# Retention with its batches' chunks in turn, its state in a ring of its own, and the first expert's layer in sixteen half tiles

## The chip, the cores and the metric

The kernel runs on one core of one Trainium2 chip. The metric is the device time of one execution in microseconds (us); a smaller number is better. Engines are named as in the profile: PE is TensorE (PEld its weight load), DVE VectorE, ACT ScalarE, POOL GpSimd, SP SyncE; a q behind a name is the queue of that engine.

## The reference, cut to what matters

Three parts follow each other. The first is a causal retention with a decay for each head, the second a mixture of 4 experts with all tokens through every expert, the third an MLP with a mish activation, which the kernel treats as experts 4 and 5.

```python
batch, n_heads, seq, head_dim = (2, 8, 576, 64)
scores = scale * np.matmul(q, k.transpose(0, 1, 3, 2))
gamma = 1.0 - 2.0 ** (-5.0 - np.arange(H, dtype=np.float32))
Dmat = np.where(rel >= 0, gamma[:, None, None] ** rel[None, :, :], 0.0)
ret = scores * Dmat[None, :, :, :]
attn = np.matmul(ret, v)                       # (2, 8, 576, 64) -> x (1152, 512)
for e in range(4):                             # w1 (512, 1024), w2 (1024, 512)
    out += p[:, e:e + 1] * (np.maximum(x @ w1[e], 0.0) @ w2[e])
g = h * np.tanh(softplus(h))                   # h = out @ w_in (512, 2048)
result = g @ w_out                             # (1152, 512)
```

## The kernel before

Retention works on 18 chunks of 64 tokens, nine for each batch, all nine of batch 0 first. A chunk lies in one of six slots of `qkv`: v and k by keys on partitions 0 to 63, k and q by features on partitions 64 to 127. For chunk c PE computes the scores of 8 heads (L448, rows 64 to 127 of the array, columns 0 to 63) and adds k times v of the chunk to the running state (L452, rows 0 to 63, columns 64 to 127): the two are issued head by head in turn and lie on opposite quarters of the array. `masked` on DVE (L822) writes the masked scores over k, POOL's `v_decay` (L1025) multiplies v in place with its decay, `state_copy` on ACT (L696, two pieces) writes the state over the next chunk's k by features, and `output` (L488) multiplies both with 128 rows at once. `decayed` on DVE (L837) takes the output out of bank 3, `first_hi` on ACT (L702) and `first_lo` on DVE (L843) split it in two fp32r parts. Since the next chunk is of the same batch, the state of chunk c has to be copied before `output(c + 1)`, and before the next state matmuls of its half (a wait inside L461).

The order on PE is written out by hand in 19 turns. Turn c holds the scores of chunk c + 1 and the state of c, then the output of chunk c - 1. The first expert's layer 1 for the first 384 tokens (8 tiles, banks 6 and 7, waits in `plain_ready`) is cut in 16 halves of two contraction steps, 6 matmuls of 384 columns each (L494 to L496). Before, a half stands behind the scores of turns 8 to 18 and another behind the output of turns 7 to 11. Matmuls on zeros (`keep_warm`, L626) stand at the start (9), behind the first scores (5) and in turns 0 (3) and 6 (8).

```python
WARM = 9
WARM_IN = {0: 3, 6: 8}
```

The weights of the experts are split by jobs: `job_hi` on ACT (L368; L364 for the sums of weight blocks, kind "s") and `job_lo` on POOL (L395; L382 to L390 for "s"). IN_TURN says in which turn a job stands; raw weights come in a ring of 8 buffers. SP issues the loads of chunks and weights in a written order with waits between them (`load_chunk`, `chunk_there`, `load_weights`). Constants come in two further loads, one on SP's queue, one on ACT's.

Behind the turns comes layer 2 of the first stage, `second(0, q)` for q from 0 to 11 with three matmuls each; it takes unit q // 3 of w2. From there on PE follows a fixed list of products and second-layer pieces for all experts, which the change doesn't touch.

## Time and profile before

| what | us |
|---|---|
| median of 3 runs | 626.67 |
| lowest and highest run | 625.93, 629.63 |
| span of the profiled execution | 625.2 |
| PE busy in that span | 618.1 |
| DVE, ACT, POOL busy | 271.6, 237.0, 285.0 |

The profiled execution is known by its span, from its first to its last instruction; the median of the runs stands 1.47 us above that. The busy time of PE is counted from modelled ends of pipelined matmuls. A few per cent of the matmul records can be missing.

### The profile page before, as it was taken

Reading aid. Unit: us, or ns where it says so; the run is one execution under the profiler, and the core shown is the slowest. Engines: PE = TensorE matmul, PEld = TensorE weight load, DVE = VectorE, ACT = ScalarE, POOL = GpSimd, SP = SyncE. Lnnn points to the kernel's source line nnn. Section 1 sums busy time; section 2 is a strip of 40 time slices with the busy share of each in tenths; the row PEclk is TensorE's granted clock in tenths of the full one; section 3 lists DMA queues with packets and bytes.
Section 4 is the critical chain, followed back from the end, with each engine's and each line's share of the span. In section 5 each row is a group of like instructions: output and inputs, shape, how many; then the busy total and the mean of one; then the engine's idle time right before and its main releaser. Section 6 shows DMA issues by size and latency. Waiting matters only on the chain.

```text
span 625.2 us, 9507 instructions
## 1 busy us (share of the span) xinstructions
PE 618.1 (99%) x3773; PEld 553.7 (89%) x3773; DVE 271.6 (43%) x388; ACT 237.0 (38%) x459; POOL 285.0 (46%) x239
## 2 busy tenths in 40 slices
PE   8999999999999999999999999999999999999997
PEld 5788899999999999999999899988989999989996
DVE  5646854433154433154433154434545432324334
ACT  3446423432223432123442223435455454334431
POOL 4657645553435542535543635532435553443300
PEclk9999999999999999999999999999999999999999
DMA  8955312332102321212312212321211233201002
GB/s 271 318 185 174 106 48 68 101 89 63 51 35 68 102 79 57 68 35 67 102 67 69 69 35 67 88 81 35 68 34 35 68 117 85 68 0 52 1 0 102
DMA packets 25147, 50.43 MB, mean 81 GB/s; under 512 B 2896, under 2 KB 3216, under 8 KB 25104
## 3 DMA queue, kind: packets, MB, share of 16 engines
q1 hardware_dynamic: 24816, 49.66, 25.4%
q8 instruction: 31, 0.51, 0.3%
q10 hardware_dynamic: 288, 0.17, 0.1%
q14 instruction: 12, 0.10, 0.0%
HBM read 47.45 MB, written 2.36 MB: 80 GB/s over the span
## 4 chain that ended last, share of the span: by engine, by line
PE 97%; DMA 1%; DVE 1%; issue 0%; ACT 0%; SPq 0%; DVEq 0%; ACTq 0%
PE bank L494 31%; PE bank L496 30%; PE bank L495 30%; PE bank L448 2%; PE bank L488 2%; DMA qkv<-in_chunks 1%; PE bank L619 1%; PE bank L452 1%; PE bank L626 0%; DVE acc_sb L895 0%; DVE acc_sb L899 0%; ACT qkv L696 0%; DVE qkv L822 0%; DVE h_lo L856 0%; SPq L418 0%
## 5 line engine op out<-in xcount | busy, mean ns | idle before, releaser
L395 POOL TENSOR_TENSOR w_lo<-w_raw,w_hi 128x512 fp32r<-128x512 f32 x96 | 132.2, 1389 | 150.7 <-ACT w_hi L368 148.9
L494 PE MATMUL bank<-w_hi,h_hi 128*128 128x512 f32 x432 | 168.8, 391 | 0.0
L496 PE MATMUL bank<-w_hi,h_lo 128*128 128x512 f32 x432 | 168.4, 390 | 0.0
L495 PE MATMUL bank<-w_lo,h_hi 128*128 128x512 f32 x432 | 168.3, 390 | 0.0
L882 DVE TENSOR_TENSOR h_act<-part,bank 128x384 f32<-128x384 f32 x96 | 52.9, 552 | 169.7 <-PE bank L496 168.9
L390 POOL TENSOR_TENSOR ws<-ws_f,ws 128x1024 fp32r<-128x1024 f32 x24 | 57.6, 2400 | 145.1 <-ACT ws L364 145.1
L496 PEld LDWEIGHTS bank<-w_hi,h_lo 128*128 128x128 f32 x432 | 81.1, 188 | 16.9
L495 PEld LDWEIGHTS bank<-w_lo,h_hi 128*128 128x128 f32 x432 | 81.1, 188 | 12.3
L494 PEld LDWEIGHTS bank<-w_hi,h_hi 128*128 128x128 f32 x432 | 81.0, 188 | 12.2
L732 ACT ACTIVATE part<-bank 128x384 f32<-128x384 f32 x72 | 35.4, 491 | 139.3 <-PE bank L496 139.3
L849 DVE SCALAR_TENSOR_TENSOR h_lo<-h_act,h_hi 128x384 fp32r<-128x384 f32 x64 | 74.3, 1170 | 20.6 <-ACT h_hi L722 20.0
L494 PE MATMUL bank<-xa_hi,w_hi 128*128 128x384 f32 x192 | 66.4, 346 | 0.0
L496 PE MATMUL bank<-xa_hi,w_lo 128*128 128x384 f32 x192 | 64.5, 336 | 0.0
L495 PE MATMUL bank<-xa_lo,w_hi 128*128 128x384 f32 x192 | 64.4, 336 | 0.0
L856 DVE TENSOR_TENSOR h_lo<-h_act,h_hi 128x384 fp32r<-128x384 f32 x48 | 38.2, 797 | 55.5 <-ACT h_hi L727 55.1
L368 ACT ACTIVATE w_hi<-w_raw 128x512 fp32r<-128x512 f32 x96 | 57.2, 618 | 0.0
L722 ACT ACTIVATE h_hi<-h_act 128x384 fp32r<-128x384 f32 x64 | 33.5, 525 | 58.5 <-DVE h_act L882 58.5
L495 PE MATMUL bank<-xt,ws 128*128 128x384 f32 x144 | 48.4, 336 | 0.0
L496 PE MATMUL bank<-xt,ws 128*128 128x384 f32 x144 | 48.4, 336 | 0.0
L494 PE MATMUL bank<-xt,ws 128*128 128x384 f32 x144 | 48.4, 336 | 0.0
L849 DVE SCALAR_TENSOR_TENSOR h_lo<-bank,h_hi 128x384 fp32r<-128x384 f32 x32 | 17.7, 554 | 59.9 <-ACT h_hi L713 59.9
L713 ACT ACTIVATE h_hi<-bank 128x384 fp32r<-128x384 f32 x32 | 15.7, 491 | 73.7 <-PE bank L496 73.7
(87 smaller groups left out, 911.4 us busy)
## 6 DMA issues: line engine op xcount, KB each, us to landing
w_raw<-in_weights SPq DMA_DIRECT2D x144, 256.0 KB, 2.8
qkv<-in_chunks SPq DMA_DIRECT2D x18, 512.0 KB, 4.6
out<-acc_sb SPq DMA_DIRECT2D x6, 256.0 KB, 2.0
out<-acc_sb SPq DMA_DIRECT2D x1, 768.0 KB, 3.6
consts<-in_consts ACTq DMA_DIRECT2D x1, 146.0 KB, 3.6
ident<-in_consts SPq DMA_DIRECT2D x1, 64.0 KB, 4.0
consts<-in_consts SPq DMA_DIRECT2D x1, 34.0 KB, 3.9
p_nat<-in_probs ACTq DMA_DIRECT2D x1, 18.0 KB, 3.6
```

Of the source, the lines that this page charges most:

```text
L368: act.activation(w_hi[int(kind == "w2")][:, x], w_raw[:, r % RAW], ACT.Copy).then_inc(s_wh, 1)
L390: pool.tensor_tensor(w_sum(x)[:, 1], ws_f[:, :], w_sum(x)[:, 0].bitcast(F32), ALU.subtract)\
L395: pool.tensor_tensor(w_lo[layer][:, x], w_raw[:, r % RAW], w_hi[layer][:, x].bitcast(F32), ALU.subtract).then_inc(s_wl, 1)
L494: pe.matmul(out, w[0], x[0], start=first, stop=False, **more)
L495: pe.matmul(out, w[0], x[1], start=False, stop=False, **more)
L496: return pe.matmul(out, w[1], x[0], start=False, stop=last, **more)
L713: act.activation(h_hi[:, tile_slot(s, i)], banks[6 + i % 2][:, 0:TC], ACT.Relu).then_inc(s_hh, 1)
L722: act.activation(h_hi[:, tile_slot(s, i)], h_act[:, i % 2], ACT.Relu).then_inc(s_hh, 1)
L732: act.activation(part[:, i], banks[6][:, 0:TC], ACT.Copy).then_inc(s_pt, 1)
L849: dve.scalar_tensor_tensor(h_lo[:, slot], full, 0.0, h_hi[:, slot].bitcast(F32), ALU.max, ALU.subtract).then_inc(s_hl, 1)
L856: dve.tensor_tensor(h_lo[:, slot], h_act[:, i % 2], h_hi[:, slot].bitcast(F32), ALU.subtract)\
L882: dve.tensor_tensor(h_act[:, i % 2], part[:, kept], banks[bank][:, 0:TC], op).then_inc(s_cc, 1)
```

## The change

Chunks alternate between the batches: chunk c is of batch c % 2 and at place c // 2 in it. Each batch has a state of its own, in bank 4 or 5. The decayed v and the copied state no longer go into `qkv` but into `sv`, a ring of four, so `state_copy` is one instruction and serves the chunk two further on. The outputs of chunks 0, 2 and 4 go to bank 6, the others to bank 3. Constants and chunk 0 come in one load on SP's queue. Weights are loaded from behind chunk 7 on. The matmuls on zeros are 7 at the start and 3 behind the first scores, and none in the turns. The sixteen halves all stand behind the output, in turns 7 to 17, in five of these turns two at a time, and the jobs' turns are written out anew. `first_lo` comes one turn later. Outside the kernel the tokens' rows are put back in order; the tables of constants are changed to match.

```diff
--- before.py
+++ after.py
...
+SLOT = 2 * HEADS * CH
+RING = 4
+
+
+def batch(c):
+    return c % BATCH
+
+
+def place(c):
+    return c // BATCH
 
 
 def has_state(c):
-    return c % PER_BATCH < PER_BATCH - 1
+    return place(c) < PER_BATCH - 1
...
-AFTER_SCORES = {8: (0, 1), 9: (1, 1), 10: (2, 1), 11: (3, 1), 12: (4, 1), 13: (5, 0), 14: (5, 1),
-                15: (6, 0), 16: (6, 1), 17: (7, 0), 18: (7, 1)}
-AFTER_OUTPUT = {7: (0, 0), 8: (1, 0), 9: (2, 0), 10: (3, 0), 11: (4, 0)}
-HIDDEN_IN = {t: c for c, (t, half) in AFTER_SCORES.items() if half}
-
-ROWS_IN = {0: 4, 1: 5, 6: 6, 7: 7, 8: 8}
-
-
-WARM_IN = {0: 3, 6: 8}
+
+
+
+HALVES_IN = {7: (0,), 8: (1, 2), 9: (3,), 10: (4,), 11: (5, 6), 12: (7, 8), 13: (9,), 14: (10, 11), 15: (12,),
+             16: (13, 14), 17: (15,)}
+ENDS_IN = {turn: half // 2 for turn, halves in HALVES_IN.items() for half in halves if half % 2}
+JOBS_IN = {6: (("w1", 0, 0),), 7: (("w1", 0, 1),), 8: (("w1", 0, 2),), 9: (("w1", 0, 3),), 10: (("w2", 0, 0),),
+           11: (("w1", 0, 4),), 12: (("w1", 0, 5),), 13: (("w2", 0, 1),), 14: (("w1", 0, 6),), 15: (("w1", 0, 7),),
+           16: (("w2", 0, 2),), 17: (("s", 0, 0),), 18: (("w2", 0, 3), ("w2", 0, 4), ("w2", 0, 5))}
+
+ROWS_IN = {5: 4, 9: 5, 11: 6, 13: 7, 15: 8}
+WARM_START, WARM_NEXT = 7, 3
...
-    for u in range(UNITS):
-        add(IN_TURN, 5 + u, "w1", 0, u)
-    for u in range(3):
-        add(IN_TURN, 12 + u, "w2", 0, u)
-    add(IN_TURN, 15, "s", 0, 0)
-    for u in range(3, 6):
-        add(IN_TURN, 13 + u, "w2", 0, u)
+    for turn, jobs in JOBS_IN.items():
+        for job in jobs:
+            add(IN_TURN, turn, *job)
...
+        sv = sb("sv", [P, RING, HEADS, DH])
...
-        ps_s = [banks[i][KEYS, :].rearrange("p (h c) -> p h c", h=HEADS) for i in range(SCORES)]
-        ps_state = [banks[i][FEATS, 0:HS * DH].rearrange("p (h c) -> p h c", h=HS) for i in range(2)]
-        ps_o = banks[3][:, 0:PAIRS * CH].rearrange("p (h c) -> p h c", h=PAIRS)
+        by_pairs = [bank[:, 0:PAIRS * CH].rearrange("p (h c) -> p h c", h=PAIRS) for bank in banks]
+        by_heads = [bank[:, :].rearrange("p (h c) -> p h c", h=HEADS) for bank in banks]
+        ps_s = [bank[KEYS] for bank in by_heads[0:SCORES]]
+        ps_state = [bank[FEATS] for bank in by_heads[4:4 + BATCH]]
...
+        def ps_o(c):
+
+            return by_pairs[6 if c < PER_BLOCK and c % 2 == 0 else 3]
...
-            load_chunk(0)
-            sp.dma_start(consts[KEYS, 0:ROW0], consts_in[KEYS, 0:ROW0]).then_inc(s_const, 16)
+            sp.dma_start(loaded[:, lead - CONSTS:lead + SLOT], first_in).then_inc(s_slot[0], 16)
             load_chunk(1)
-
-            for c in range(2, 6):
-                if c > 2:
-                    chunk_there(c - 3)
-                load_chunk(c)
-            for u in range(UNITS):
-                chunk_there(3 + u)
-                load_weights(u)
-                chunk_there(4 + u)
-                load_chunk(6 + u)
-            for c in range(6 + UNITS, CHUNKS):
+            load_chunk(2)
+            for c in range(3, 8):
                 chunk_there(c - 3)
                 load_chunk(c)
-                load_weights(UNITS + c - 6 - UNITS)
-            sp.dma_start(ident[:, :], consts_in[:, CONSTS:]).then_inc(s_id, 16)
-            for r in range(UNITS + CHUNKS - 6 - UNITS, len(LOADS)):
+            for c in range(8, CHUNKS):
+                chunk_there(c - 2)
+                load_weights(c - 8)
+                load_chunk(c)
+            sp.dma_start(ident[:, :], ident_in).then_inc(s_id, 16)
+            for r in range(CHUNKS - 8, len(LOADS)):
...
-                return pe.matmul(ps_state[h // HS][:, h % HS], by_keys(c, 1)[:, h], by_keys(c, 0)[:, h],
-                                 start=(c % PER_BATCH == 0 and h % HS == 0), stop=True, skip_group_check=True)
+                return pe.matmul(ps_state[batch(c)][:, h], by_keys(c, 1)[:, h], sv[KEYS, c % RING, h],
+                                 start=(place(c) == 0 and h == 0), stop=True, skip_group_check=True)
...
+                    if place(c) > 0:
+                        pe.wait_ge(s_st, states(c - BATCH))
                 for h in range(HEADS):
-                    if has_state(c) and c > 0 and h % HS == 0:
-                        pe.wait_ge(s_st, 2 * states(c - 1) - 1 + h // HS)
...
-                if c % PER_BATCH > 0:
+                if place(c) > 0:
                     rows = slice(0, P)
-                    pe.wait_ge(s_st, 2 * states(c - 1))
-                if c > 0:
+                    pe.wait_ge(s_st, states(c - BATCH))
+                if c >= PER_BLOCK:
                     pe.wait_ge(s_xt, c)
+                elif c > 1:
+                    pe.wait_ge(s_xt, c - 1)
                 for hp in range(PAIRS):
                     for x in range(2):
-                        mm = pe.matmul(ps_o[DH * x:DH * (x + 1), hp], qkv[rows, c % SLOTS, 0, 2 * hp + x],
+                        mm = pe.matmul(ps_o(c)[DH * x:DH * (x + 1), hp], sv[rows, c % RING, 2 * hp + x],
                                        qkv[rows, c % SLOTS, 1, 2 * hp + x], start=True, stop=True)
...
-            keep_warm(WARM)
+            keep_warm(WARM_START)
             pe.wait_ge(s_slot[0], landed(0))
             for h in range(HEADS):
                 mm = scores_head(0, h)
             mm.then_inc(s_sc, 1)
-            keep_warm(5)
+            keep_warm(WARM_NEXT)
             for c in range(TURNS):
                 if c < CHUNKS:
                     scores_and_state(c)
-                if c in AFTER_SCORES:
-                    plain_half(*AFTER_SCORES[c])
-                keep_warm(WARM_IN.get(c, 0))
                 if c > 0:
                     output(c - 1)
-                if c in AFTER_OUTPUT:
-                    plain_half(*AFTER_OUTPUT[c])
+                for half in HALVES_IN.get(c, ()):
+                    s, i = divmod(half // 2, ITEMS)
+                    if half % 2 == 0:
+                        plain_ready(s, i)
+                    plain_products(s, i, range(KH * (half % 2), KH * (half % 2 + 1)))
...
-                act.wait_ge(s_sc, c + 2)
+
                 act.wait_ge(s_kv, states(c))
-                for i in range(2):
-                    at = by_feats(c + 1, 0)[:, HS * i:HS * (i + 1)]
-                    act.activation(at, ps_state[i], ACT.Copy).then_inc(s_st, 1)
+                if c >= BATCH:
+                    act.wait_ge(s_o, c - BATCH + 1)
+                act.activation(sv[FEATS, (c + BATCH) % RING], ps_state[batch(c)], ACT.Copy).then_inc(s_st, 1)
...
+                if c - 1 in ENDS_IN:
+                    plain_hi(*divmod(ENDS_IN[c - 1], ITEMS))
                 if c < CHUNKS and has_state(c):
                     state_copy(c)
-                for t, at in HIDDEN_IN.items():
-                    if at == c:
-                        plain_hi(t // ITEMS, t % ITEMS)
...
+                    plain_lo(*divmod(ENDS_IN[c - 1], ITEMS))
                 if c < CHUNKS:
                     masked(c)
+                if c > 1 and c != PER_BLOCK + 1:
+                    first_lo(c - 2)
                 if c > 0:
                     decayed(c - 1)
                 if c in ROWS_IN:
                     rows(ROWS_IN[c])
-                for t, at in HIDDEN_IN.items():
-                    if at == c:
-                        plain_lo(t // ITEMS, t % ITEMS)
-                if c > 0:
+                if c == PER_BLOCK:
                     first_lo(c - 1)
+            first_lo(CHUNKS - 1)
...
-                v = by_keys(c, 0)
-                pool.tensor_tensor(v, v, key_decay[KEYS, c % PER_BATCH].unsqueeze(2).broadcast_to([CH, HEADS, DH]),
+                if c >= RING:
+                    pool.wait_ge(s_o, c - RING + 1)
+                pool.tensor_tensor(sv[KEYS, c % RING], by_keys(c, 0),
+                                   key_decay[KEYS, place(c)].unsqueeze(2).broadcast_to([CH, HEADS, DH]),
                                    ALU.mult).then_inc(s_vd, 1)
...
-                    pool.wait_ge(s_xl, c)
+                    if c > 1:
+                        pool.wait_ge(s_xl, c - 1)
...
+        "first": np.concatenate([tables(), chunks[0].reshape(P, SLOT)], axis=1),
+        "chunks": chunks[1:],
+        "ident": np.eye(P, dtype=np.float32),
+        "probs": moe_domain_probs.reshape(BATCH, PER_BATCH, CH, MOE_EXPERTS).transpose(0, 2, 1, 3).reshape(P, -1),
...
-    nc = bacc.Bacc("TRN2", target_bir_lowering=False, num_devices=1)
+    nc = bacc.Bacc("TRN2", target_bir_lowering=False, num_devices=1, dynamic_dma_scratch_size=1024)
```

## Rows read from the trace of the kernel before

**Rows 1.** The stage table: busy time per engine, clock, DMA share, GB/s.

```profile
0.00:25.79 25.79, 22.08 (x410) 15.53 (x410) 13.68 (x30) 9.46 (x24) 11.67 (x15) 1.00 0.87 292
25.79:62.20 36.41, 36.41 (x549) 31.06 (x545) 21.75 (x42) 19.86 (x49) 25.92 (x24) 1.00 0.59 200
62.20:625.20 563.00, 559.59 (x2824) 507.07 (x2820) 236.16 (x318) 207.69 (x389) 247.44 (x201) 1.00 0.21 63
```

**Rows 2.** Who waited for whom, TensorE, whole span: total, times, longest.

```profile
PE bank L626 <- issue: 1.1, 1, 1.1
PE bank L448 <- DMA qkv<-in_chunks: 0.6, 1, 0.6
PE bank L448 <- ACT qkv L696: 0.4, 2, 0.2
```

**Rows 3.** The chain that ended last, turns 5 and 6: start, duration, what.

```profile
18.70 0.62 PE bank L488 x16
19.32 0.24 PE bank L448
...
20.47 0.97 PE bank L626 x4
21.44 1.07 issue
22.51 1.04 PE bank L626 x4
```

**Rows 4.** The same chain, turns 10 and 11, and the second layer.

```profile
38.41 0.38 PE bank L494
...
38.96 0.17 PE bank L496
...
39.66 0.20 PE bank L448
...
40.74 0.38 PE bank L494
...
41.99 0.61 PE bank L488 x16
...
62.93 0.23 PE bank L496
```

**Rows 5.** TensorE in order of time, start of the program.

```profile
1.31 3.64 PE L626 MATMUL bank<-zeros 128*128 128x512 bf16 x9 [1.31 <-POOL zeros L1019]
...
5.95 1.25 PE L626 MATMUL bank<-zeros 128*128 128x512 bf16 x5
7.79 0.27 PE L448 MATMUL bank<-qkv 64*64 64x64 f32 x1 [0.58 <-DMA qkv<-in_chunks]
```

**Rows 6.** VectorE, ScalarE and GpSimd in order of time, after output 5.

```profile
24.28 0.42 DVE L837 TENSOR_TENSOR x_tmp<-bank,row_decay 128x256 f32<-128x256 f32 x1 [2.90 <-PE bank L488]
```

```profile
24.74 0.42 ACT L702 ACTIVATE xa_hi<-x_tmp 128x256 fp32r<-128x256 f32 x1 [3.21 <-DVE x_tmp L837]
25.07 0.61 ACT L368 ACTIVATE w_hi<-w_raw 128x512 fp32r<-128x512 f32 x1
```

```profile
25.82 1.30 POOL L395 TENSOR_TENSOR w_lo<-w_raw,w_hi 128x512 fp32r<-128x512 f32 x1 [2.37 <-ACT w_hi L368]
```

**Rows 7.** ScalarE and GpSimd in order of time, end of the retention.

```profile
59.98 1.06 ACT L364 ACTIVATE ws<-ws_f 128x1024 fp32r<-128x1024 f32 x1 [0.54 <-POOL ws_f L387]
60.94 0.61 ACT L368 ACTIVATE w_hi<-w_raw 128x512 fp32r<-128x512 f32 x1
```

```profile
61.18 2.39 POOL L390 TENSOR_TENSOR ws<-ws_f,ws 128x1024 fp32r<-128x1024 f32 x1 [1.23 <-ACT ws L364]
63.53 4.61 POOL L395 TENSOR_TENSOR w_lo<-w_raw,w_hi 128x512 fp32r<-128x512 f32 x3
```

**Rows 8.** GpSimd in order of time, its wait for chunk 7.

```profile
18.75 1.10 POOL L1025 TENSOR_TENSOR qkv<-qkv,consts 64x512 f32<-64x512 f32 x1 [0.73 <-DMA qkv<-in_chunks]
```

**Rows 9.** DMA queues from 20 to 22.6 us: packets, MB, share.

```profile
q8 instruction: 1, 0.02, 2.2%
```

More of the change, by code:

```diff
@@ L37 @@
 RAW = 8
-WARM = 9
 MASK0 = PER_BATCH * HEADS
@@ L179, with build @@
 SUM_JOBS = [i for i, job in enumerate(JOBS) if job[0] == "s"]
-def build(nc, chunks_in, consts_in, probs_in, weights_in, out):
+def build(nc, first_in, chunks_in, ident_in, probs_in, weights_in, out):
     with ExitStack() as ctx:
@@ L522, in plain_products @@
                     mm.then_inc(s_l1, 1)
-            def plain_half(t, half):
-                s, i = divmod(t, ITEMS)
-                if half == 0:
-                    plain_ready(s, i)
-                plain_products(s, i, range(2 * half, 2 * half + 2))
             def product(s, j):
@@ L830, in decayed @@
             def decayed(c):
-                i = c % PER_BATCH
+                i = place(c)
                 if i > 0:
@@ L935, in _ @@
                               ALU.mult).then_inc(s_pc, 1)
-            dve.wait_ge(s_rows, 16)
+            dve.wait_ge(s_pc, 4)
+            dve.wait_ge(s_slot[0], landed(0))
             for i in range(1, 4):
                 rows(i)
-            dve.wait_ge(s_const, 16)
-            dve.wait_ge(s_pc, 4)
             for c in range(TURNS):
+                if c - 1 in ENDS_IN:
+                    plain_lo(*divmod(ENDS_IN[c - 1], ITEMS))
                 if c < CHUNKS:
                     masked(c)
+                if c > 1 and c != PER_BLOCK + 1:
+                    first_lo(c - 2)
                 if c > 0:
@@ L1023, in v_decay @@
                 pool.wait_ge(s_slot[c % SLOTS], landed(c))
-                v = by_keys(c, 0)
-                pool.tensor_tensor(v, v, key_decay[KEYS, c % PER_BATCH].unsqueeze(2).broadcast_to([CH, HEADS, DH]),
+                if c >= RING:
+                    pool.wait_ge(s_o, c - RING + 1)
+                pool.tensor_tensor(sv[KEYS, c % RING], by_keys(c, 0),
+                                   key_decay[KEYS, place(c)].unsqueeze(2).broadcast_to([CH, HEADS, DH]),
                                    ALU.mult).then_inc(s_vd, 1)
-            pool.wait_ge(s_const, 16)
+            pool.wait_ge(s_slot[0], landed(0))
             v_decay(0)
@@ L1047, in tables @@
     c = np.arange(PER_BATCH, dtype=np.float64)
-    consts = np.zeros((P, CONSTS + P))
+    consts = np.zeros((P, CONSTS))
     keys = gamma[None, None, :] ** (MID - CH * c[None, :, None] - i[:, None, None])
     consts[KEYS, 0:MASK0] = keys.reshape(CH, MASK0)
-    consts[KEYS, MASK0:ROW0] = i[:, None] <= i[None, :]
+    consts[:, MASK0:ROW0] = np.tile(i[:, None] <= i[None, :], (2, 1))
     rows = gamma[:, None] ** (i[None, :] - MID) / np.sqrt(DH)
@@ L1076 @@
     weights = [halves(moe_w1[e], moe_w2[e]) for e in range(MOE_EXPERTS)] + [halves(moe2_w_in, moe2_w_out)]
+    chunks = np.concatenate([np.stack([by_tokens(v), by_tokens(k)], axis=2),
+                             np.stack([by_features(k), by_features(q)], axis=2)], axis=1)
     arrays = {
[L1078 to L1081 removed]
+        "first": np.concatenate([tables(), chunks[0].reshape(P, SLOT)], axis=1),
+        "chunks": chunks[1:],
+        "ident": np.eye(P, dtype=np.float32),
+        "probs": moe_domain_probs.reshape(BATCH, PER_BATCH, CH, MOE_EXPERTS).transpose(0, 2, 1, 3).reshape(P, -1),
         "weights": np.concatenate(weights),
@@ L1088 @@
     build(nc, *args, out)
-    return run(nc, [{f"in_{n}": a for n, a in arrays.items()}], core_ids=[0]).results[0]["out"]
+    rows = run(nc, [{f"in_{n}": a for n, a in arrays.items()}], core_ids=[0]).results[0]["out"]
+    return np.ascontiguousarray(rows.reshape(PER_BATCH, BATCH, CH, DM).transpose(1, 0, 2, 3).reshape(TOKENS, DM))
```

29 lines of the change are left out of this document (11 added, 18 removed).

## The prediction

> **What bounds the kernel now.** I read the stage table first [rows 1]: from 62.20 us on PE is busy 559.59 of 563.00 us, and from 25.79 to 62.20 all of the time; only ahead of 25.79 does it have idle time, 3.7 us of it. The change leaves the work behind 62.20 as it is, so the question is when PE gets there. Next I read who PE waits for [rows 2]: the waits that the change addresses, for the copied state, are 0.4 us in total; waiting for chunk 1 costs 0.6 and a wait for nothing that the profile shows 1.1. So idle time is not where the gain lies. What fills PE is read from the chain: 0.97 + 1.07 + 1.04 = 3.08 us in turn 6 are matmuls on zeros and the gap amid them [rows 3]. The granted clock is 1.00 in all three stretches [rows 1].
>
> **Prices on PE.** Without a half tile a turn costs 19.32 to 20.47 for scores and state, 1.15 us, and 0.62 for the output, 1.77 in all [rows 3]. In a turn with halves: a half from 38.41 to 39.66 and from 40.74 to 41.99 is 1.25, scores and state 39.66 to 40.74 are 1.08, the output 0.61 [rows 4]. Six matmuls at the even pace inside a half, 0.17 for one [rows 4], would be 1.04, so the change of kind on both sides of a half costs 0.21. The change makes no matmul of the retention cheaper: scores and state already lie on two quarters at once before.
>
> **The halves.** Before, from the first half to layer 2: 16 halves x 1.25 + 9 score groups (turns 8 to 16) x 1.08 + 11 outputs (chunks 7 to 17) x 0.62 = 36.5; the trace has 36.41 [rows 1]. After, they stand in 11 groups, so 11 x 1.25 + 5 x 1.04 = 18.95, with 9.72 and 6.82 unchanged: 35.5. That is a gain of 1.0, bounded by 0 (switches cost the same) and 1.1.
>
> **The start.** The first load grows from 512 KB to 726 KB (428 more columns of 4 bytes on 128 partitions) and takes in the two loads of constants, 180 KB. SP's queue has one issue fewer ahead of chunk 1. Before, chunk 1 landed just ahead of 7.79 and PE had waited 0.58 for it [rows 5]. Bytes are nearly the same; small pieces go. I take turn 0 at 7.1, between 6.5 and 8.0 (0.2 later if only the bytes count). PE has time for it: 7 + 3 matmuls on zeros take less than the 9 + 5 did (3.64 and 1.25 [rows 5]).
>
> **Turns 0 to 6.** Turn 0 is 1.08, the next five 1.77 each if nothing waits: turn 6 begins at 7.1 + 1.1 + 8.85 = 17.0 against 19.32 [rows 3]. The state wait is now for a copy two turns old, hidden behind a whole turn; if that cover went, it would cost the 0.2 a turn that it does now. The 3 zero matmuls of turn 0 (some 0.75 in the chain) go too. Chunks: the core moved 292 GB/s over the first 25.79 us [rows 1], 1.8 us for a chunk of 524 KB, so the loads can just keep up; chunk 7, wanted at 17.0, landed at 18.7 before [rows 8] behind 4 chunks and 3 weights issued in between, and weights now stand behind it. Chunks 2 to 7 one after another from 7.1 on would end at 17.9, 0.9 late; but chunk 2 is issued at the start too and is well under way when chunk 1 lands. Price if they can't keep up: 0 to 1.5; I take 0.
>
> **To the first half.** It needs the low part of chunk 5 and the low part of the first weight, job w1 0, now in turn 6 instead of 5. The way there is in [rows 6]: output 5 ended at 24.17 (23.55 + 0.62), then x_tmp 24.28, x_hi 24.74, w_hi 25.07 and w_lo 25.82 to 27.12, 2.95 us in all; before, that weight was the second one and PE did not wait for it. After, output 5 ends at 17.0 + 1.77 = 18.8, DVE has `first_lo(4)` ahead of `decayed(5)` (some 0.4 later), so w_lo is there at 18.8 + 0.4 + 2.95 = 22.1. PE has only turn 7's 1.7 us to do and waits some 1.6. Queued behind the waiting half are the scores of turn 8, and behind them masks, state copies and `v_decay`; nothing of it is needed sooner. The gap of 1.07 us: one transfer of 0.02 MB on an instruction queue runs between 20 and 22.6 [rows 9]. If it returns ahead of output 5's end the whole way moves by 1.07, if behind, it hides in the wait. I take half, 0.5: first half at 22.6, between 21.9 and 24.0, against 25.79.
>
> **Layer 2.** It begins at 22.6 + 35.5 = 58.1 instead of 62.20. Here a cover goes. Unit 3 of w2 is wanted by the tenth of twelve pieces, 27 matmuls x 0.23 [rows 4] = 6.2 us in: 64.3 (68.4 before). Its split stands behind that of the weight sums: ACT's 1.06 us, POOL's 2.39, then 1.34 to 1.54 for w2 3 [rows 7], and before it was there at about 64.9, 3.5 us early. Now ACT can start L364 behind `first_hi(17)`, which follows output 17 (58.1) by 1.6 (tile 7's low part 0.55, a low part, `decayed` 0.42, the copy 0.31): 59.7 + 1.06 + 0.1 + 2.39 + 1.5 = 64.8. PE waits 0.5, bounds 0 and 1.5. `second` of unit 3 and all products stand behind it. The low parts of x for the products and the sums `xs_a`, `xs_b` move up with output 17 and keep some 3 us of slack. Moving SP's weight loads back costs nothing there: ten of them are issued by chunk 17's time, each 0.8 us of bandwidth, in turns of 2.95 to 4.0 us. The waits for the ring `sv` (output c - 2 ahead of `v_decay(c + 2)` and of `state_copy(c)`) are for a turn that is over, 0 to 0.1. `state_copy` as one instruction saves ACT 0.03 a turn, off the path.
>
> **Sum.** 62.20 - 58.1 = 4.1, less 0.5: 3.6 us of gain at the end of the list. The profiled span 625.2 gives 621.6. The median stands 1.47 above its span; 626.67 - 3.6 = **623.1 us**. It splits into 2.3 (start, state waits and turn 0's zeros), 0.9 (turn 6 to first half), 1.0 (fewer groups), less 0.5, the rest rounding. Ends: turn 0 at 6.5, no gap, no wait for w2 3 give a gain of 5.2 (621.5); turn 0 at 8.0, a gap of 1.07 and a wait of 1.5 give 1.2 (625.5). With the scatter of the medians (three runs spread over 3.7 us) I go a little beyond on both sides.
>
> **Rivals.** (A) *Transfers take the wait's place.* Chunks come as late as before (chunk 7 at 18.7 [rows 8]); turn 6 begins at 18.9, the first half at 24.5, and 35.5 more makes 60.0, where w2 3 is no longer late: a gain of 2.2, 624.5. For it: 0.87 DMA share [rows 1]. Against: fewer bytes are asked for ahead of chunk 7. Chance 0.2, inside the range.
> (B) *Slower, by PE's clock.* The zeros that go stood where PE had nothing to do. The first nine took 3.64, 0.40 each, the next five 0.25 each [rows 5]: 512 columns take 0.43 at 1.2 GHz and 0.21 at 2.4, so the engine began at the lower level, and the higher came while it ran them. With 7, PE falls idle from about 4.3 until the first load lands near 5, and again ahead of turn 0 and of the first half (1.6 us). If the faster level is not granted until the halves run, each turn costs up to 3.54 instead of 1.77; the gain is used up from the second such turn on, and turns 0 to 6 together would cost 12 us less the 1 us wait they hide: about 634. Against: before, PE idled 0.58 and 1.07 and the clock stayed at 1.00. Chance 0.06. The Trainium skill (TensorE: Matmul & The Clock Gate, What's actually happening) says that the throttled state is the default and activity releases it, which speaks against removing zeros; the sum by it is this rival's.
> (C) *More than forecast*: w1 0 lands on PE without a wait and w2 3 in time; first half at 20.5, layer 2 at 56.0: a gain of 6.2, 620.5. It needs the 2.95 us way to shrink by half. Chance 0.04.
> (D) *It does not do what it says*: the waits moved elsewhere, the halves in pairs wait for their bank (`h_lo` of two tiles before) or weight, as w1 1 does, split one turn after w1 0: 16 halves spread as before, gain 0 to 1, 626. Chance 0.1.
> The forecast itself has 0.6.
>
> **Chances.** A measurement of this kernel can tell about 1% (6.3 us) from no change. Over 1% faster means under 620.4: 0.07. Over 1% slower means over 632.9, only (B): 0.05. Range 620.8 to 626.8; it holds the forecast with (A) and (D), and leaves out (B) and (C) and a little on either side.
>
> **What would show it.** Turn 0's first scores near 7.1; score groups 1.77 apart up to turn 6; one PE gap of 1 to 2 us ahead of the first L494, ended by w_lo L395; 11 groups of halves, 35.5 us from the first to layer 2; one wait of some 0.5 us about 6 us into it, ended by w_lo; behind it the list as long as before, 563.0. Granted clock 1.00 throughout. The prediction is wrong if PE waits for POOL or DVE between halves, if the first records of the turns are twice as far apart, or if the stretch behind the start of layer 2 is longer.

## The result and the profile after

| what | before | after |
|---|---|---|
| median, 8 runs each on one chip | 626.81 | 629.94 |
| lowest and highest run | 625.70, 629.63 | 627.99, 630.71 |
| span of the profiled execution | 625.2 | 628.8 |
| first half / layer 2 begins / rest of the span | 25.79 / 62.20 / 563.0 | 25.63 / 62.09 / 566.7 |

The ratio of after to before is 1.0046, interval 1.0029 to 1.0062: slower by 0.46% or 2.9 us, where 3.6 us of gain was forecast. The profiled execution of after took 630.63, 1.8 above its span; in the other profiled executions it is 1.7 to 2.1, so spans can be compared. The level of TensorE's clock is told in two ways below. The column of the granted clock shows a drop in the middle of a run, but reads 1.00 at the start of every run here, also where the matmuls go at half their pace. At the start the level is therefore read from the pace: 0.49 us for a matmul on zeros at the lower level and about 0.25 at the higher.

The stage table of after, in the columns of [rows 1], with a short stretch at the end:

```profile
0.00:25.63 25.63, 20.65 (x395) 16.09 (x395) 16.67 (x29) 9.25 (x17) 11.67 (x16) 1.00 0.74 252
25.63:62.09 36.46, 35.51 (x544) 31.29 (x544) 22.57 (x41) 17.74 (x37) 24.41 (x21) 1.00 0.69 228
62.09:628.70 566.61, 560.21 (x2824) 506.95 (x2820) 239.21 (x318) 209.45 (x390) 253.56 (x204) 1.00 0.21 63
12.00:15.00 3.00, 3.00 (x108) 3.00 (x105) 2.00 (x4) 1.60 (x3) 1.52 (x2) 1.00 0.31 94
```

The same last stretch of before:

```profile
12.00:15.00 3.00, 2.82 (x84) 2.53 (x79) 2.37 (x5) 1.60 (x5) 2.14 (x2) 1.00 0.90 303
```

Layer 2 begins where it did (0.1 us earlier instead of 4.1), and the work behind it, which the change leaves alone, takes 3.6 us more. Up to the end of the last matmul it is 563.2 instead of 559.8; the rest of the span, with the last results on their way out, is 3.5 instead of 3.2. PE does as many matmuls there; the idle time in it is 6.4 us instead of 3.4. The waits say where. PE's waits in after, whole span (total, times, longest; before in [rows 2]):

```profile
PE bank L498 <- POOL w_lo L404: 2.4, 2, 1.6
PE bank L623 <- POOL zeros L1015: 1.3, 1, 1.3
PE bank L450 <- DMA loaded<-in_first: 1.2, 1, 1.2
PE bank L450 <- DMA loaded<-in_chunks: 1.2, 2, 1.0
PE bank L498 <- ACT part L728: 1.2, 1, 1.2
PE bank L492 <- DVE xf L832: 0.8, 1, 0.8
PE bank L492 <- issue: 0.5, 2, 0.3
```

**Behind layer 2** PE waits twice. TensorE in order of time:

```profile
70.08 0.50 PE L498 MATMUL bank<-w_hi,h_hi 128*128 128x512 f32 x1 [1.57 <-POOL w_lo L404]
...
80.18 0.44 PE L498 MATMUL bank<-xt,ws 128*128 128x384 f32 x1 [1.17 <-ACT part L728]
```

The second is the end of a chain of four. VectorE, then GpSimd, then ScalarE, same stretch:

```profile
65.74 3.16 DVE L958 TENSOR_TENSOR xs_a<-xf,xs_a 128x768 f32<-128x768 f32 x1
...
74.72 2.04 DVE L920 TENSOR_TENSOR xt<-xs_a,xt 128x768 fp32r<-128x768 f32 x1
76.68 2.05 DVE L920 TENSOR_TENSOR xt<-xs_b,xt 128x768 fp32r<-128x768 f32 x1
78.66 0.54 DVE L877 TENSOR_TENSOR h_act<-part,bank 128x384 f32<-128x384 f32 x1
```

```profile
64.99 3.09 POOL L399 TENSOR_TENSOR ws<-ws_f,ws 128x1024 fp32r<-128x1024 f32 x1 [1.24 <-ACT ws L373]
68.05 9.86 POOL L404 TENSOR_TENSOR w_lo<-w_raw,w_hi 128x512 fp32r<-128x512 f32 x5
```

```profile
79.23 0.52 ACT L718 ACTIVATE h_hi<-h_act 128x384 fp32r<-128x384 f32 x1 [5.22 <-DVE h_act L877]
79.66 0.47 ACT L728 ACTIVATE part<-bank 128x384 f32<-128x384 f32 x1
```

VectorE in before, the same instructions, behind the first two sums:

```profile
64.94 2.05 DVE L959 TENSOR_TENSOR xs_a<-xf 128x768 f32<-128x768 f32 x1
66.92 2.04 DVE L960 TENSOR_TENSOR xs_b<-xf 128x768 f32<-128x768 f32 x1
...
72.59 0.95 DVE L925 TENSOR_TENSOR xt<-xs_a,xt 128x768 fp32r<-128x768 f32 x1
73.46 0.95 DVE L925 TENSOR_TENSOR xt<-xs_b,xt 128x768 fp32r<-128x768 f32 x1
74.41 0.56 DVE L882 TENSOR_TENSOR h_act<-part,bank 128x384 f32<-128x384 f32 x1
```

The subtraction of a low part of `xt` takes 2.04 us in place of 0.95, while POOL's `w_lo` takes 9.86 / 5 = 1.97 in place of 1.30 [rows 6] and its `ws` 3.09 in place of 2.39 [rows 7]. In after they lie side by side; in before POOL stood idle from 68.1 to 73.5 us. DVE's last subtraction there starts 0.04 us ahead of POOL's next and keeps its 0.95, and POOL's split then takes 2.06. Before has the price in its own trace: its first two sums lie beside POOL's `w_lo` (63.53 to 68.14 [rows 7]) and take 2.05 and 2.04, and the six instructions of the same size behind them take 0.94 to 0.96. In after six of the eight are slow, and the eight take 15.0 us in sum instead of 9.8. So `h_act`, which stands behind them on DVE, begins at 78.66 instead of 74.41, behind it ACT's `h_hi` and `part`, and behind that PE.

**Ahead of layer 2.** TensorE in order of time, start of after:

```profile
1.31 3.17 PE L623 MATMUL bank<-zeros 128*128 128x512 bf16 x7 [1.31 <-POOL zeros L1015]
5.69 1.97 PE L450 MATMUL bank<-loaded 64*64 64x64 f32 x16 [1.20 <-DMA loaded<-in_first]
7.59 1.46 PE L623 MATMUL bank<-zeros 128*128 128x512 bf16 x3
8.98 0.36 PE L450 MATMUL bank<-loaded 64*64 64x64 f32 x1
9.14 0.31 PE L450 MATMUL bank<-loaded 64*64 64x64 f32 x1
9.25 0.31 PE L450 MATMUL bank<-loaded 64*64 64x64 f32 x1
```

The three zeros take 0.49 each (0.25 in [rows 5]) and the scores stand 0.11 apart; at 23 us they stand 0.06 apart. PE is at the lower of its levels until 12.2 us, near the end of turn 0. It had idled 1.20 us for the first load, but that alone does not explain it: e6 idles 0.96 and has the higher level at 4.1 us, e3 and e10 do not idle there and have it only at 10.1 and 10.4 us. Turn 0 begins at 8.98 instead of the forecast 7.1, and output 0 ends at 13.0, in before at 11.2. That output frees the slot for chunk 6, so the DMA engines are busy for a third of the stretch from 12 to 15 us (share 0.31, before 0.90), chunk 8 is late for turn 7 (PE waits 1.02 for it, in e6 0.99 but 2.5 us earlier), and POOL decays it before it comes to the first weight. TensorE, then GpSimd:

```profile
23.08 0.27 PE L450 MATMUL bank<-loaded 64*64 64x64 f32 x1 [1.02 <-DMA loaded<-in_chunks]
...
25.63 0.44 PE L498 MATMUL bank<-xa_hi,w_hi 128*128 128x384 f32 x1 [0.78 <-POOL w_lo L404]
```

```profile
23.11 1.03 POOL L1022 TENSOR_TENSOR sv<-loaded 64x512 f32<-64x512 f32 x1 [2.27 <-DMA loaded<-in_chunks]
24.16 1.41 POOL L404 TENSOR_TENSOR w_lo<-w_raw,w_hi 128x512 fp32r<-128x512 f32 x1
```

### The profile page after: what moved, and what is told of

The parts are those of the page before. It is cut to its first block, busy times and chain, and to the rows that moved or that the text cites. A ratio compares the mean times of both kernels' runs of the same rounds, so it can differ in the third digit from the quotient of the medians.

```text
span 628.8 us, 9463 instructions
## 1 busy us (share of the span) xinstructions
PE 616.4 (98%) x3758; PEld 554.3 (88%) x3758; DVE 278.4 (44%) x388; ACT 236.4 (38%) x443; POOL 289.6 (46%) x239
## 4 chain that ended last, share of the span: by engine, by line
PE 90%; DVE 5%; DMA 2%; ACT 1%; issue 1%; POOL 1%; SPq 0%; DVEq 0%; POOLq 0%
PE bank L498 29%; PE bank L500 29%; PE bank L499 29%; DMA loaded<-in_chunks 2%; PE bank L450 1%; DVE xt L920 1%; DVE xb_lo L838 1%; DMA loaded<-in_first 1%; PE bank L616 1%; DVE xs_a L958 0%; PE bank L492 0%; POOL w_lo L404 0%; DVE loaded L817 0%; DVE xf L832 0%; DVE acc_sb L890 0%
## 5 line engine op out<-in xcount | busy, mean ns | idle before, releaser
L404 POOL TENSOR_TENSOR w_lo<-w_raw,w_hi 128x512 fp32r<-128x512 f32 x96 | 134.5, 1414 | 143.9 <-ACT w_hi L377 143.9
```

Source lines behind the costliest of these rows:

```text
L404: pool.tensor_tensor(w_lo[layer][:, x], w_raw[:, r % RAW], w_hi[layer][:, x].bitcast(F32), ALU.subtract).then_inc(s_wl, 1)
```

## The experiments

All compute the whole reference. Each was timed in rounds with the kernel before on the same chip; ratios are to that one. "First half / layer 2 / rest" are landmarks of the profiled span. "Low clock" counts the runs whose mean granted clock over the span is below 0.9985, that is with a stretch at the lower level somewhere behind the start; the start itself doesn't show in it. The six profiled runs that are low (e2, e5, e8, e9, e12 and e13) each have one such stretch.

| kernel | base | first half / layer 2 / rest | median | ratio (95%) | low clock |
|---|---|---|---|---|---|
| after | | 25.63 / 62.09 / 566.7 | 629.94 | 1.0046 (1.0029 to 1.0062) | 3 of 8 |
| e1 | after | 23.70 / 59.34 / 566.7 | 628.99 | 1.0026 (1.0009 to 1.0043) | 3 of 12 |
| e2 | after | 24.43 / 63.59 / 565.4 | 629.14 | 1.0026 (1.0011 to 1.0041) | 5 of 12 |
| e3 | after | 24.71 / 62.20 / 565.4 | 628.81 | 1.0026 (1.0010 to 1.0042) | 5 of 12 |
| e4 | before | 25.44 / 61.88 / 566.1 | 631.10 | 1.0057 (1.0037 to 1.0076) | 5 of 8 |
| e5 | after | 24.48 / 64.12 / 565.0 | 631.87 | 1.0073 (1.0051 to 1.0095) | 6 of 6 |
| e6 | after | 23.28 / 58.92 / 565.0 | 627.57 | 1.0004 (0.9988 to 1.0020) | 4 of 12 |
| e7 | before | 23.15 / 59.53 / 563.1 | 627.50 | 0.9997 (0.9975 to 1.0020) | 6 of 12 |
| e8 | after | 23.65 / 64.15 / 564.6 | 630.62 | 1.0056 (1.0040 to 1.0072) | 6 of 6 |
| e9 | after | 24.40 / 61.19 / 565.1 | 627.01 | 0.9997 (0.9983 to 1.0011) | 3 of 12 |
| e10 | after | 25.77 / 61.50 / 566.9 | 628.55 | 1.0019 (1.0003 to 1.0035) | 4 of 12 |
| e11 | after | 24.73 / 60.40 / 566.6 | 629.34 | 1.0037 (1.0022 to 1.0051) | 0 of 12 |
| e12 | after | 24.09 / 59.77 / 570.0 | 631.96 | 1.0090 (1.0067 to 1.0113) | 6 of 6 |
| e13 | after | 23.79 / 60.36 / 569.1 | 632.37 | 1.0087 (1.0066 to 1.0109) | 6 of 6 |
| e14 | before | 24.29 / 60.68 / 563.0 | 625.89 | 0.9986 (0.9970 to 1.0002) | 0 of 12 |

Of 100 runs of the kernel before, 2 were low. The rest of e10 holds 5.0 us behind the last matmul, where all other profiled runs have 3.2 to 3.5; up to the last matmul e6, e9 and e10 agree (561.7 to 561.9), and so do before, e7 and e14 (559.8 to 559.9) and after, e1 and e11 (563.1 to 563.2).

### First four: the start, and the splits' turns

e1, the zeros at the start as before:

```diff
-WARM_START, WARM_NEXT = 7, 3
+WARM_START, WARM_NEXT = 9, 5
```

> The changed kernel with 9 and 5 matmuls on zeros again in place of 7 and 3. Theory S (the lower TensorE clock at the start delays output 0, with it the load of chunk 6, and so turn 7 and the first half): the clock rises near 4.4 us instead of 12.2, turn 0 begins near 7.9, the first half near 23 instead of 25.6, and since the splits behind the turns hang on output 17, the whole is 2 to 3 us shorter than the changed kernel, near 627. Theory L alone (the late splits on GpSimd and VectorE's sums slow each other behind layer 2's start): the first half may come earlier, but the waits of 1.6 and 1.2 us stay as long or grow by what was gained, so the time stays within 1 us of the changed kernel's.

e2, weight sums and w2 3 to 5 split earlier:

```diff
-JOBS_IN = {6: (("w1", 0, 0),), 7: (("w1", 0, 1),), 8: (("w1", 0, 2),), 9: (("w1", 0, 3),), 10: (("w2", 0, 0),),
-           11: (("w1", 0, 4),), 12: (("w1", 0, 5),), 13: (("w2", 0, 1),), 14: (("w1", 0, 6),), 15: (("w1", 0, 7),),
-           16: (("w2", 0, 2),), 17: (("s", 0, 0),), 18: (("w2", 0, 3), ("w2", 0, 4), ("w2", 0, 5))}
+JOBS_IN = {6: (("w1", 0, 0),), 7: (("w1", 0, 1),), 8: (("w1", 0, 2),), 9: (("w1", 0, 3),), 10: (("w1", 0, 4),),
+           11: (("w1", 0, 5),), 12: (("w2", 0, 0),), 13: (("w1", 0, 6),), 14: (("w1", 0, 7), ("w2", 0, 1)),
+           15: (("w2", 0, 2),), 16: (("w2", 0, 3), ("s", 0, 0)), 17: (("w2", 0, 4),), 18: (("w2", 0, 5),)}
```

To make room it moves the jobs of turns 10 to 15 too: w1 4 to 7 stand a turn earlier, w2 0 two turns and w2 1 one turn later.

> The changed kernel with the splits of w2 3, of the weight sums and of w2 4 moved from turns 17 and 18 to 15, 16 and 17; 7 and 3 zeros stay. Theory L: the wait for w_lo (1.6 us) and the wait for part (1.2 us) behind layer 2's start go, 2.5 to 3.2 us shorter than the changed kernel, near 627. Theory S alone: nothing is won, since these waits would only follow from the late start; within 0.7 us of the changed kernel. A rival within L: splits in turns 14 to 16 delay v_decay or first_lo, and PE waits there for 1 us or more instead.

e3 is both:

> Both edits together. If S and L are separate causes the gains add: 4.5 to 6 us shorter than the changed kernel, 624 to 625.5, below the kernel before. If L only absorbs what S gives, it is as e2. If chunk transfers bound the turns whatever the clock does, the first half stays at 24.5 or later and the time is near 626.

e4 is the kernel before with its splits as late as after's:

```diff
-    add(IN_TURN, 15, "s", 0, 0)
+    add(IN_TURN, 17, "s", 0, 0)
...
-        add(IN_TURN, 13 + u, "w2", 0, u)
+        add(IN_TURN, 18, "w2", 0, u)
```

> The kernel before with the split of the weight sums in turn 17 instead of 15 and w2 3 to 5 all in turn 18. Theory L: VectorE's sums and low parts of xt take 2 us each instead of 1, PE waits for w_lo and for part, 2 to 3.5 us longer than the kernel before. If the late splits do not matter by themselves: within 0.5 us of the kernel before.

e4 is the clean one: nothing of the retention is changed, layer 2 begins at 61.88, and the rest grows by 3.1 us. TensorE and VectorE of e4:

```profile
71.08 0.50 PE L494 MATMUL bank<-w_hi,h_hi 128*128 128x512 f32 x1 [2.78 <-POOL w_lo L395]
```

```profile
71.77 2.04 DVE L925 TENSOR_TENSOR xt<-xs_b,xt 128x768 fp32r<-128x768 f32 x1
```

So the loss behind layer 2 is the late splits', and the slow subtractions come with them. In e1 the matmuls go at the higher pace from 6.2 us on instead of 12.2, the first half is at 23.70, and from there to layer 2 it is 35.64, but the rest is still 566.7. e3 has the same nine and five zeros, and its higher pace comes only at 10.1 us (first half at 24.71), so these zeros do not settle when it comes. e2 and e3 lose ahead of layer 2 what they save behind it: from the first half to layer 2 e3 takes 37.49, with 2.0 us of waits for `decayed`, for a reason that e5 shows larger. e2 takes 39.16, and part of that is clock. Its profiled run is one of its five low ones:

```profile
23.40:30.00 6.60, 5.80 (x61) 4.94 (x58) 2.00 (x5) 1.73 (x4) 4.27 (x4) 0.50 0.93 318
```

PE had waited 1.87 us for chunk 8 up to 21.79, and waits 0.80 more for `w_lo` up to the first half. In the kernel before, eight zeros stand in turn 6, just ahead of this stretch.

So e1 stayed within 1 us of after, as theory L has it, e2 and e3 missed what was expected (near 627 and 624 to 625.5), and e4 lost 3.7 us, a little more than the 2 to 3.5 of theory L, by a longer wait for `w_lo` and none for `part`.

### e5: sums in turn 15

Turns 10 to 14 are those of e2. Against after:

```diff
-JOBS_IN = {6: (("w1", 0, 0),), 7: (("w1", 0, 1),), 8: (("w1", 0, 2),), 9: (("w1", 0, 3),), 10: (("w2", 0, 0),),
-           11: (("w1", 0, 4),), 12: (("w1", 0, 5),), 13: (("w2", 0, 1),), 14: (("w1", 0, 6),), 15: (("w1", 0, 7),),
-           16: (("w2", 0, 2),), 17: (("s", 0, 0),), 18: (("w2", 0, 3), ("w2", 0, 4), ("w2", 0, 5))}
+JOBS_IN = {6: (("w1", 0, 0),), 7: (("w1", 0, 1),), 8: (("w1", 0, 2),), 9: (("w1", 0, 3),), 10: (("w1", 0, 4),),
+           11: (("w1", 0, 5),), 12: (("w2", 0, 0),), 13: (("w1", 0, 6),), 14: (("w1", 0, 7), ("w2", 0, 1)),
+           15: (("s", 0, 0),), 16: (("w2", 0, 2), ("w2", 0, 3)), 17: (("w2", 0, 4),), 18: (("w2", 0, 5),)}
```

> The changed kernel with the weight sums' job in turn 15, w2 2 and 3 in 16, w2 4 in 17, w2 5 in 18. In the run with the sums in turn 16 (e2) ScalarE waited for GpSimd's four adds with tile 7 queued behind, and VectorE's sums began at 68.2 us. Theory L (where the splits stand decides what follows layer 2's start): the adds are done by 57 us, VectorE's sums begin near 65, the waits for w_lo and for part go, and the part behind layer 2's start is 563 to 563.5 us as in the kernel before (566.7 in the changed kernel, 565.4 in e2); the median is 2.5 to 3.5 us below the changed kernel's, near 627. Rival: the waits are only moved into the turns, and the time stays within 1 us of e2's 629.1.

A miss. ScalarE, VectorE and TensorE of e5:

```profile
58.05 1.06 ACT L373 ACTIVATE ws<-ws_f 128x1024 fp32r<-128x1024 f32 x1 [1.47 <-POOL ws_f L396]
59.02 1.13 ACT L377 ACTIVATE w_hi<-w_raw 128x512 fp32r<-128x512 f32 x2
60.17 0.49 ACT L709 ACTIVATE h_hi<-bank 128x384 fp32r<-128x384 f32 x1
```

```profile
60.70 0.56 DVE L844 SCALAR_TENSOR_TENSOR h_lo<-bank,h_hi 128x384 fp32r<-128x384 f32 x1 [4.46 <-ACT h_hi L709]
61.17 0.67 DVE L817 TENSOR_TENSOR loaded<-bank,loaded 64x512 f32<-64x512 f32 x1
```

```profile
63.50 0.69 PE L492 MATMUL bank<-loaded,sv 128*64 128x64 f32 x16 [3.99 <-DVE xf L832]
```

ACT waits in its order for the sums that POOL is still adding; `h_hi` of a tile stands behind that, DVE's `h_lo` behind `h_hi`, the masks and `decayed` behind `h_lo`, and PE behind them. The wait is in a queue, not for data that PE wants. Just behind it the clock falls; a stretch of e5:

```profile
64.60:67.80 3.20, 3.20 (x9) 2.43 (x8) 2.79 (x6) 0.83 (x2) 1.71 (x2) 0.50 0.72 225
```

### e6: POOL splits w2 6 and 7 only behind DVE's low parts

```diff
+            pool.wait_ge(s_tl, 4)
             for s in range(1, ALL_STAGES):
                 for job in IN_STAGE.get(s, ()):
                     job_lo(pool, job)
```

> The changed kernel with one wait more: GpSimd splits w2 6 and 7 only when VectorE's four low parts of xt are done. Contention theory (GpSimd's w_lo and VectorE's low parts of xt each take 2.0 us when they meet and 1.3 and 0.95 when they don't): the last of the low parts of xt fall from 2.04 to 0.95 us, the 1.2 us wait for part is gone or under 0.3, and the part behind layer 2's start shrinks from 566.7 by about 1.2; the wait for w2 3 (1.6) stays. Rival (VectorE is slow there for another reason, such as its strided reads): L920 stays at 2 us and the time does not fall.

Stage table, VectorE, GpSimd and TensorE of e6:

```profile
23.28:58.92 35.64, 35.49 (x544) 31.28 (x544) 21.77 (x43) 17.93 (x37) 24.02 (x21) 1.00 0.69 232
58.92:623.80 564.88, 559.92 (x2824) 506.96 (x2820) 236.77 (x318) 209.45 (x390) 251.21 (x204) 1.00 0.21 63
```

```profile
69.58 2.05 DVE L920 TENSOR_TENSOR xt<-xs_b,xt 128x768 fp32r<-128x768 f32 x1
71.55 0.95 DVE L920 TENSOR_TENSOR xt<-xs_a,xt 128x768 fp32r<-128x768 f32 x1
72.42 0.95 DVE L920 TENSOR_TENSOR xt<-xs_b,xt 128x768 fp32r<-128x768 f32 x1
```

```profile
73.44 2.85 POOL L404 TENSOR_TENSOR w_lo<-w_raw,w_hi 128x512 fp32r<-128x512 f32 x2 [2.64 <-DVE xt L920]
```

```profile
66.92 0.50 PE L498 MATMUL bank<-w_hi,h_hi 128*128 128x512 f32 x1 [1.58 <-POOL w_lo L404]
```

One added wait on POOL turns the same instruction from 2.05 to 0.95 us within one trace, at the moment POOL is held. PE's wait for `part` is gone, the wait for w2 3 is not, the rest is 565.0 instead of 566.7 (561.7 instead of 563.2 up to the last matmul), and the median falls by 2.4 us; the two intervals do not overlap. A DVE instruction and one of POOL that each have two inputs in SBUF slow each other. The Trainium skill (SBUF — State Buffer, Who interferes with whom) has it that a DVE instruction with two SBUF inputs contends with a GpSimd instruction that reads SBUF. The trace agrees that they contend, and shows both sides longer, 2.05 for 0.95 and 1.97 for 1.30.

### e7: the old order with few zeros

```diff
-WARM = 9
+WARM = 7
...
-WARM_IN = {0: 3, 6: 8}
+WARM_IN = {}
...
-            keep_warm(5)
+            keep_warm(3)
```

> The kernel before with 7 and 3 matmuls on zeros and none in turns 0 and 6. Clock theory (zeros where PE has nothing to do keep or bring TensorE's clock): the clock rises later than 4.4 to 6.2 us in the profile, some runs show a mean granted clock of 0.997 or less (1 in 31 of the kernel before do), and the median is 1 to 3 us above the kernel before. If the zeros only filled time: the same median within 0.5 us, or up to 1 us shorter, since turn 6 loses 3 us of zeros but waits for the first weights.

```profile
23.15:59.53 36.38, 36.38 (x545) 31.02 (x545) 21.60 (x42) 19.28 (x47) 25.85 (x24) 1.00 0.64 214
59.53:622.50 562.97, 559.62 (x2824) 507.05 (x2820) 236.07 (x318) 207.71 (x389) 247.35 (x201) 1.00 0.21 63
```

This stage table is the most telling one. Without any of the restructuring the old kernel reaches layer 2 at 59.53, 2.67 us earlier than before; all of the change, with an early clock, reaches it at 58.92 (e6). So in these traces the zeros are 2.67 of the gain ahead of layer 2 and the rest of the change 0.6. Each is one profiled run, and those of e6 and e7 are the fastest of their twelve, which that of before is not. Six runs of e7 have a low clock, with a median of 628.92, against 626.77 of the other six, and these six are only 0.8 under the 627.54 of before in the same rounds. Low clocks are 6 of 12 here and 1 of 23 in before, so the zeros do hold the clock; which of the fifteen that e7 takes out do it, this run does not say. The median stayed where it was, against the 1 to 3 us more that were expected: the others win what the low runs lose.

### e8 to e13: towards a better version

e8 is e5 with e6's wait, 12 and 5 zeros at the start, 3 in turn 6 and 4 in turn 7:

> e5 and e6 together with more zeros: 12 at the start, 5 behind the first scores, 3 in turn 6 and 4 in turn 7 ahead of the first half. If the changed kernel's gain was eaten by the clock at the start and by the late splits, this one has it: first half near 23, layer 2 at 58.5 to 59.5, 563 behind it, 624 to 625.5 in the median and few runs with a mean granted clock under 0.9985. If chunk transfers or the splits' chain bound the turns anyway: 626.5 or more.

In the profiled run PE's wait of 4.0 us for `decayed` came again, and with it the drop; all six runs are low. More zeros ahead of it don't prevent that.

e9 is e6 with w2 3 ahead of the sums:

```diff
-           16: (("w2", 0, 2),), 17: (("s", 0, 0),), 18: (("w2", 0, 3), ("w2", 0, 4), ("w2", 0, 5))}
+           16: (("w2", 0, 2),), 17: (("w2", 0, 3), ("s", 0, 0)), 18: (("w2", 0, 4), ("w2", 0, 5))}
```

> The changed kernel with the wait of e6 and the split of w2 3 ahead of the weight sums in turn 17. Theory (w2 3 is late because it stands behind the sums' 1.1 and 2.4 us): the 1.6 us wait goes, the part behind layer 2's start is 563 to 563.6 us, the median 1 to 2 us below e6's 627.6. Rival: the sums or w2 4 become late in turn, and PE waits there for as long; same time as e6.

The wait for w2 3 is gone (0.3 left for `w_lo` in the whole span) and `part` is late again by 1.2: with the sums later, w2 4 and 5 fall on DVE's subtractions. The profiled run is one of the three low ones, and no wait in it is over 1.3 us. TensorE's level fell ahead of the first half, behind 0.67 us without a releaser and 1.08 for chunk 8:

```profile
21.50:24.70 3.20, 3.20 (x49) 2.96 (x50) 1.10 (x3) 0.96 (x2) 3.20 (x3) 0.50 0.80 266
```

The jobs of e9 are those of after up to turn 16, and its zeros too. The rest is 565.1, not the 563 to 563.6 expected.

e10 is e9 with 9 and 5 zeros at the start, 3 in turn 0 and 5 in turn 7:

> As e9, with 9 and 5 zeros at the start, 3 in turn 0 and 5 in turn 7 ahead of the first half. Clock theory: fewer of its runs have a mean granted clock of 0.997 or less than e9's (4 in 12 in e6), and the spread shrinks; the zeros in turn 0 cost 0.7 us at most, those in turn 7 lie in the wait for w1 0. Median 624.5 to 626. Rival: the clock falls elsewhere (behind a wait among the halves) and the share stays at a third; then it is as e9 or up to 1 us longer.

A miss: 25.77 for the first half, as slow as after, and 4 of 12 low. The higher pace came only at 10.4 us, in turn 0, behind 14 zeros. The four low runs are no slower than the others here (628.4 against 628.8).

e11 is after with all zeros of before, in their places (ahead of the output):

```diff
+WARM_IN = {0: 3, 6: 8}
-WARM_START, WARM_NEXT = 7, 3
+WARM_START, WARM_NEXT = 9, 5
```

> The changed kernel with all zeros of the kernel before: 9, 5, 3 in turn 0, 8 in turn 6. Clock theory: the share of runs with a mean granted clock under 0.9985 falls from 3 in 8 towards the 2 in 54 of the kernel before; the span of the best runs grows by 1 to 3 us against the changed kernel's best (626.1) for the zeros themselves. If the waits behind layer 2's start (1.6 and 1.2 us) are what lets the clock fall, the share stays at a third or more, with the median near 630 to 631.

None of twelve runs is low, against 3 of 8; but the rest is still 566.6 and the median 629.34, so most of after's loss against before (1.0037 of 1.0046) is there with the clock held. Its zeros take time of their own, yet layer 2 begins 1.8 us earlier than in before. e12 is e11 and e9 with a further wait ahead of w2 4; e13 the same with 7 and 3 zeros and none in the turns:

```diff
+                    if c == CHUNKS:
+                        pool.wait_ge(s_tl, 4)
```

> All zeros of the kernel before (9, 5, 3, 8) and, against the waits behind layer 2's start, w2 3 split ahead of the sums and w2 4 to 7 only behind VectorE's four low parts of xt. If contention of GpSimd with VectorE is the whole of the 3.7 us that the changed kernel is longer behind layer 2's start, that part is 563.0 to 563.5 us; if the zeros hold the clock, no more than 1 run in 12 has a mean granted clock under 0.9985. Layer 2 at 60.4 as in e11: median 625.5 to 626.5, 1 us under the kernel before. If something else makes the part long (the banks, the order of the splits), it stays at 565.

> The same waits and order with the changed kernel's 7 and 3 zeros. Clock theory: best runs 1.5 to 2.5 us below e12's best (near 624), but 3 to 5 of 12 runs with a mean granted clock under 0.9985, and a wider spread; median between 625 and 627. If the zeros only cost time: as tight as e12 and 1.5 us shorter.

TensorE and the stage table of e12:

```profile
74.45 0.79 PE L499 MATMUL bank<-w_hi,h_hi 128*128 128x512 f32 x1 [4.12 <-POOL w_lo L405]
```

```profile
74.40:80.00 5.60, 5.54 (x14) 4.68 (x15) 0.41 (x1) 0.00 (x0) 5.60 (x7) 0.50 0.56 147
```

All four subtractions take 0.95 now, as expected. But w2 4 is 4.1 us late for PE, the rest is 570.0 and all six runs are low, in e13 too. I had mis-sized when PE wants it. Holding POOL back works only for weights that nobody is near to needing; here w2 4 is, w2 6 and 7 are not.

### e14: the kernel before with four zeros in turn 6

```diff
-WARM_IN = {0: 3, 6: 8}
+WARM_IN = {6: 4}
```

> The kernel before with 4 zeros in turn 6 in place of 8 and none in turn 0. The start has 2.7 us to give (layer 2 began at 59.5 without any, 62.2 with all); with four it should begin near 60.5. If four are enough to hold the clock, at most 1 run in 12 has a mean granted clock under 0.9985 and the median is 625.5 to 626.5; if not, a third of the runs and the median of the kernel before.

Layer 2 begins at 60.68, near the 60.5 expected, and the rest is 563.0 as in before. The lowest median of all, 625.89 against 626.54 in the same rounds, none of twelve low; its ratio of 0.9986 reaches to 1.0002, so a gain of 0.1% is not shown. Seven of before's zeros can go without a low run in twelve: those of turn 0 and four of the eight in turn 6.

## Why the prediction was wrong

**The step that failed** in every profile with after's split order is in the part on layer 2: "the low parts of x for the products and the sums `xs_a`, `xs_b` move up with output 17 and keep some 3 us of slack". I costed POOL's late splits as a wait of PE for POOL alone. They also lie beside DVE's sums and subtractions and can double them, as before's own first two sums show, so that DVE came to `h_act` at 78.66, 4.25 later than before although layer 2 began at the same time. That took the slack and 1.17 us of PE. e4 shows the slow subtractions in the old kernel, e6 takes the wait away in the new one. None of my rivals had this mechanism.

**The wait for w2 3** was priced 0.5 with an end at 1.5 and measured 1.57: the mechanism was right, its terms too short, for the same reason (2.39 for `ws` became 3.09, 1.5 for a split 1.97). The two waits, 2.7 us together, are most of the 3.6 by which the stretch behind layer 2 grew, where 0.5 was in the sum. The prediction also says that only the stretch ahead of 25.79 has idle time; [rows 1] has 3.4 us behind 62.20 as well.

**Turn 0 at 7.1** failed in the profiled run: 8.98, beyond the end of 8.0. I sized it by transfers and said that PE had time for its zeros; at the lower level it had not. Rival B had this cause, but placed its price in turns 1 to 6, named the gap ahead of the first half as a second place, and thought it decisive only from the second turn; one turn at the lower level was enough, because SP's loads hang on output 0. With the higher level early, e6 has 7.16 for turn 0, near the 7.1, and 23.28 for the first half, inside 21.9 to 24.0. This rests on a comparison of profiled runs, not on an edit that moves the level alone. When the level rises differs from one profiled run to the next, also of like starts: 4.1 us in e6, 9.7 in e2, 12.2 in after, with 7 and 3 zeros each; by 5.0 in e11, at 6.2 in e1 and at 10.1 and 10.4 in e3 and e10, with 9 and 5. I have no run that says what decides it.

**Eleven groups in 35.5 us** held: 35.64 in e1 and in e6, 35.73 in e10. In after it was 36.46, with 0.95 us of idle time, 0.81 of it one wait for `xf`.

**The gap of 1.07 us** is not there in that size; gaps with no releaser are 0.3 at most in after. Its place was forecast well: by the prediction's count of 22 records fewer it would fall in the last third of output 5, and there it is in after, ahead of the last six of 16 matmuls:

```profile
21.67 0.39 PE L492 MATMUL bank<-loaded,sv 128*64 128x64 f32 x6 [0.25 <-issue]
```

The place moves with the matmuls ahead of it, as a fixed place in PE's list would: with four zeros more (e1) it is ahead of the last ten, with seven more (e8, e10) ahead of the last thirteen. It is 0.45 to 0.67 us there and in e5 and e9, 1.07 in before and e4, and e2, e3, e6 and e13 show none there; what sets the size is open. The first half waits for `w_lo`, as forecast, 0.78 instead of some 1.6, since PE itself came late.

**The split of the gain** was wrong in what it credits. I put 2.3 on the start, state waits and turn 0's zeros, 0.9 on turn 6 and 1.0 on fewer groups. e7's profile gets 2.67 by fewer zeros alone, in the old order. And these zeros are not free to take: low clocks are 3 of 8 in after and 6 of 12 in e7, but 2 of 100 in before and none of 24 in e11 and e14.

**As a sum**: forecast +4.1 ahead of layer 2 and -0.5 behind; the profile has +0.1 and -3.6. Of the 4.0 missing ahead, 3.2 is not missing in e6 (58.92 against 62.09): 2.35 of it at the first half, which goes with the late start, and 0.8 in the halves, which does not (e10 starts as late and has 35.73, e9 starts early and has 36.79). The other 0.8 is forecast too much. Of the 3.1 too much behind, e6's one wait on POOL gives back 1.7.

**Still open**: where in the three low runs of after the clock fell, since its profiled run has no such stretch. The two low profiled runs without a long wait, e2 and e9, have it around the first half, where before has its eight zeros; that makes this the likely place in after, and no run shows it. So it is open too how much of the 2.9 us is clock. By e11 (none low, 1.0037) most of the ratio is there without it, within intervals of 0.0015 to either side.
